# Gathered rows in a ring of two, one transpose per tile for four matmuls, in a top-32 attention and two-layer mixture-of-experts kernel

## The chip, the cores and the metric

One Trainium2 chip, one core of it. The metric is device time in microseconds (us) of one execution of the whole program. Three runs of the kernel before gave 1107.25, 1108.45 and 1108.89 us; the median, 1108.45 us, is what the change is measured against. Engine names: PE is TensorE's matmul, PEld its weight load, DVE is VectorE, ACT is ScalarE, POOL is GpSimd, SP is SyncE (it issues DMAs here).

## The reference

Three layers run one after the other. The change touches only the last one.

```python
# 1. attention over (4, 8, 576, 64): scores, only the 32 largest of a row are kept, softmax, times v
# 2. soft mixture of experts on x = (2304, 512): 8 experts with 4 slots each
#    d = softmax(x @ phi, over tokens); slot_out = relu((d.T @ x) @ w1[e]) @ w2[e]
#    x = softmax(x @ phi, over slots) @ slot_out            # every row is a mix of 32 rows
# 3. top-2 mixture of experts on that x
logits = x @ w_gate
noisy_logits = logits + np.log1p(np.exp(x @ w_noise)) * noise
top2 = np.argpartition(-noisy_logits, 2, axis=1)[:, :2]
top2_w = softmax of the two chosen logits
for e in range(8):
    for k in range(2):
        mask = top2[:, k] == e
        h = np.maximum(x[mask] @ w1[e], 0.0)                # 512 -> 1024
        out[mask] += top2_w[mask, k, None] * (h @ w2[e])    # 1024 -> 512
```

Since layer 2 makes each row of x a combination of 32 slot rows with weights c (one row of 32 numbers per token), the kernel never forms x for layer 3. It multiplies slot rows and w1 once per expert (a matrix `g_sb[e]`), and a token needs only its 32 combination weights, already scaled by its gate.

## The kernel before, in words

The first 780 us are attention, the soft layer and the routing. Routing ends with a table in DRAM, `xs_rows`: for each of the 4608 (token, choice) pairs a row of 32 numbers, and with a list in SBUF, `list_i`, which gives for each of up to 44 tiles of 128 pairs the row numbers to gather and the output rows to add to. The tiles are sorted by expert. With this input there are 40 tiles, five for most experts.

The last stage, from about 794 us, is a software pipeline over these tiles. Each engine runs a hardware loop per expert with bounds read from a table (`tile_bounds`), and semaphores tie the engines together. For tile i:

- POOL holds the indices of a tile in two small buffers `now[0]` and `now[1]` (`fetch`, line 1349, a copy of two numbers per partition: gather index and output index), gathers the 128 rows of 32 numbers from DRAM into the single buffer `x_in` (`gather`, line 1354, an indirect DMA) and adds the finished outputs to DRAM (line 1373, an indirect DMA with add). In one turn of its loop it fetches indices, waits for the output copy (`f_yc`), issues the scatter, waits until TensorE has read `x_in` (`f_t`), issues the gather, and then waits until the scatter has landed (`f_out`).
- PE, `f_trans` (line 776): four matmuls with `x_in` as 32 columns of weights and the identity as moving operand. They write the transposed rows four times, one above the other, into one PSUM bank. It waits for the gather (`x_ready`). This is done one tile ahead: it stands behind the first-layer matmuls of the tile before.
- ACT, `c_high` (line 947) copies that bank to `cs`, rounded to fp32r, and DVE, `c_low` (line 1233) turns the lower half of `cs` into the rounding remainder.
- PE, line 794: eight matmuls of `g_sb[e]` and `cs` (layer one of the expert). ACT, line 960: two Relu into `h_hi`. DVE, line 1250: the remainder `h_lo`.
- PE, lines 805 and 810: 16 and 8 matmuls with 512 columns each (layer two), with `w2_hi`, `w2_lo` and `h_hi`, `h_lo`. The first of them waits for the Relu (`f_hc`) and for `f_yc`, that is until DVE has copied the output of the tile before out of the bank (line 1237).
- Between experts ACT makes `w2_high` of the weights of a coming expert (line 926, two instructions), DVE makes `w2_low` (line 1207, two instructions), and ACT issues the DMA that loads 2 MB of weights for experts 4 to 7 (line 375, at the start of experts 1 to 4). Behind the first expert ACT also copies `g_sb` 6 and 7 (line 920).

Each engine executes its own queue in order, so the order of the work is what the loops write down, and an instruction that waits holds back all behind it on its engine.

## Time and profile before

| | us |
|---|---|
| median of the three runs | 1108.45 |
| the profiled execution | 1109.94 |
| its span | 1108.1 |
| PE busy | 939.6 (85%) |
| ACT busy | 617.3 (56%) |
| DVE busy | 817.3 (74%) |
| POOL busy | 708.6 (64%) |
| 40 turns of the tile loop | about 794 to 1108.1 |

The profiled execution took 1.5 us more than the median of the others. The busy shares are averages over stages with different limits: in the first 750 us DVE, ACT and POOL are busy together, and in the last 310 us PE is busy nearly all the time while the others have long gaps. The profile's chain of waits says the same for its last stretch: it runs along PE, lines 805, 810, 794 and 776, with breaks at a few places.

### The profile page before, as it was taken

What the parts mean: (1) busy time and instruction counts of PE and PEld (TensorE: products, weight loads), DVE (VectorE), ACT (ScalarE), POOL (GpSimd) and SP (SyncE); (2) the same over time, 40 slices, a digit from 0 to 9 for tenths busy, and PEclk for the clock granted to TensorE, in tenths of its full rate; (3) what the DMA queues carried; (4) which work ended last, traced back from release to release, by engine and by line L of the source; (5) the groups of instructions that cost most, each with busy time, mean ns of one, the idle gap of its engine ahead of it and who ended that gap; (6) DMA issues with size and microseconds to landing.
All of it is one profiled execution on the core that took longest, in us unless ns stands there. A gap on an engine that the chain in (4) does not pass through costs nothing.

```text
span 1108.1 us, 20890 instructions
## 1 busy us (share of the span) xinstructions
PE 939.6 (85%) x6032; PEld 639.7 (58%) x6032; DVE 817.3 (74%) x1870; ACT 617.3 (56%) x1199; POOL 708.6 (64%) x900
## 2 busy tenths in 40 slices
PE   3888888888888888888888897865699999899995
PEld 1655555555555555555555574222387787788884
DVE  6999999999999999999999964008525442444331
ACT  5888887788878877878888841102414331231110
POOL 2798989899899899899899851002234344344443
PEclk9999999999999999999999988966899999899998
DMA  9911011011011011011001007899524534433332
GB/s 352 390 46 35 11 45 44 0 44 44 0 44 44 0 44 44 0 44 44 30 14 44 0 1 290 351 421 425 236 30 106 116 50 104 109 40 40 40 41 31
DMA packets 21585, 105.12 MB, mean 95 GB/s; under 512 B 2944, under 2 KB 4016, under 8 KB 12464
## 3 DMA queue, kind: packets, MB, share of 16 engines
q1 hardware_dynamic: 13696, 84.54, 19.4%
q0 software_dynamic: 7136, 11.20, 7.7%
q10 hardware_dynamic: 720, 8.98, 2.2%
q8 instruction: 17, 0.28, 0.1%
q14 instruction: 16, 0.13, 0.0%
HBM read 88.37 MB, written 16.07 MB: 94 GB/s over the span
## 4 chain that ended last, share of the span: by engine, by line
DVE 39%; PE 29%; issue 22%; DMA 5%; ACT 2%; DVEq 2%; POOL 1%; SPq 0%; ACTq 0%; POOLq 0%; PEldq 0%
PE psum L805 12%; DVE arena L996 10%; DVE arena L1003 8%; PE psum L810 5%; DVE arena L992 5%; DVE arena L1009 3%; DVE arena L980 3%; DVE arena L984 2%; DMA arena<-w_soft 2%; DVE arena L988 2%; PE psum L794 2%; DMA arena<-xs_rows,arena 2%; DVE arena L1000 2%; DVE w_lo L1207 1%; PE psum L523 1%
## 5 line engine op out<-in xcount | busy, mean ns | idle before, releaser
L1289 POOL TENSOR_SCALAR arena<-arena 128x576 bf16<-128x576 f32 x142 | 246.7, 1738 | 55.4 <-DVE arena L1009 27.9
L564 PE MATMUL psum<-arena 128*128 128x130 f32 (+3 forms) x1600 | 227.9, 284 | 0.2 <-ACT arena L855 0.2
L564 PEld LDWEIGHTS psum<-arena 128*128 128x128 f32 (+3 forms) x1600 | 187.3, 180 | 43.2 <-ACT arena L855 13.6
L523 PE MATMUL psum<-arena 64*128 64x288 f32 (+1 forms) x640 | 112.0, 461 | 98.2 <-DVE arena L988 93.8
L1298 POOL TENSOR_TENSOR arena<-arena 128x576 f32<-128x576 f32 x142 | 178.6, 1277 | 0.0
L960 ACT ACTIVATE h_hi<-psum 128x512 fp32r<-128x512 f32 x80 | 43.6, 596 | 217.6 <-PE psum L794 217.6
L836 ACT ACTIVATE arena<-psum,arena 128x576 bf16<-128x576 f32 x144 | 106.6, 740 | 91.7 <-DVE arena L980 91.7
L1237 DVE COPY arena<-psum 128x512 f32 x41 | 28.3, 691 | 166.9 <-PE psum L810 156.6
L805 PE MATMUL psum<-w_hi,h_hi 128*128 128x512 f32 x320 | 135.6, 424 | 5.5 <-DVE arena L1237 2.8
L805 PE MATMUL psum<-w_lo,h_hi 128*128 128x512 f32 x320 | 130.0, 406 | 0.0
L523 PEld LDWEIGHTS psum<-arena 64*128 64x128 f32 (+1 forms) x640 | 44.3, 179 | 146.5 <-DVE arena L988 119.8
L839 ACT ACTIVATE arena<-arena 128x576 bf16<-128x576 bf16 x144 | 111.6, 775 | 4.7
L984 DVE MAX8 arena<-psum 128x8 f32<-128x576 f32 x144 | 108.8, 755 | 5.9 <-PE psum L535 5.8
L846 ACT ACTIVATE arena<-arena 128x576 f32<-128x576 f32 x144 | 112.2, 779 | 0.0
L829 ACT COPY arena<-psum 128x576 f32<-128x576 f32 x144 | 91.7, 637 | 35.9 <-PE psum L523 35.9
L1373 POOL DMA_INDIRECT out<-arena x40 | 63.8, 1595 | 73.7 <-PE psum L776 69.6
L1003 DVE MAX8 arena<-arena 128x8 f32<-128x576 f32 x144 | 107.2, 745 | 0.0
L988 DVE MATCH_REPLACE8 arena<-arena,psum 128x576 f32<-128x576 f32 x144 | 106.8, 741 | 0.0
L980 DVE MAX8 arena<-arena 128x8 f32<-128x576 f32 x144 | 106.0, 736 | 0.1
L992 DVE MAX8 arena<-arena 128x8 f32<-128x576 f32 x144 | 106.0, 736 | 0.0
L996 DVE MATCH_REPLACE8 arena<-arena 128x576 f32<-128x576 f32 x144 | 106.0, 736 | 0.0
L550 PE MATMUL psum<-arena 128*128 128x128 f32 x576 | 92.0, 284 | 2.8 <-POOL arena L1298 2.8
(192 smaller groups left out, 1602.8 us busy)
## 6 DMA issues: line engine op xcount, KB each, us to landing
weights<-w_soft SPq DMA_DIRECT2D x21, 1024.0 KB, 17.0
arena<-qkv SPq DMA_DIRECT2D x15, 1189.0 KB, 5.3
weights<-w_top SPq DMA_DIRECT2D x12, 1024.0 KB, 27.2
arena<-w_soft SPq DMA_DIRECT2D x11, 1024.0 KB, 12.1
weights<-w_top SPq DMA_DIRECT2D x3, 2048.0 KB, 18.9
weights<-w_top ACTq DMA_DIRECT2D x3, 2048.0 KB, 7.7
out<-arena SPq DMA_DIRECT2D x1, 4864.0 KB, 18.3
arena<-w_top SPq DMA_DIRECT2D x4, 1024.0 KB, 27.7
```

What stands on the lines that cost most here:

```text
L523: last = nc.tensor.matmul(bank(2 * (t % 2) + x, SH)[q0:q0 + rows, :], qT[u][half, w * P + q0:w * P + q0 + rows], kT[u][half, h * SH:(h + 1 ...
L564: last = nc.tensor.matmul(o_place(n, k)[0:rows, :], wT[0:kr, t % 2, kc, q0:q0 + rows], v_, start=(kc == 0), stop=(kc == KC - 1))
L805: nc.tensor.matmul(bank(B_Y), h_hi[:, f, :], w[:, f, :], start=(f == 0 and part_ == 0), stop=False)
L846: nc.scalar.activation(e_sb[t % S_SLOTS], s_sb[t % S_SLOTS], ACT.Exp, bias=nmax[n % 3][:, x:x + 1], scale=SCALE).then_inc(expd, 1)
L980: nc.vector.max(top(t, 0), s_sb[t % S_SLOTS]).then_inc(top8, 1)
L984: nc.vector.max(top(t, 1), scores_of(t)).then_inc(top16, 1)
L988: nc.vector.match_replace(by_half(work[t % 2]), top(t, 1), scores_of(t), NEG).then_inc(struck16, 1)
L992: nc.vector.max(top(t, 2), work[t % 2]).then_inc(top24, 1)
L996: nc.vector.match_replace(work[t % 2], top(t, 2), work[t % 2], NEG).then_inc(struck24, 1)
L1003: nc.vector.max(top(t, 3), work[t % 2]).then_inc(top32, 1)
L1289: nc.gpsimd.tensor_scalar(keep[t % 2], s_sb[t % S_SLOTS], kth_sb[:, t % S_SLOTS:t % S_SLOTS + 1], None, ALU.is_ge) \
L1298: nc.gpsimd.tensor_tensor(e_sb[t % S_SLOTS], e_sb[t % S_SLOTS], keep[t % 2], ALU.mult) \
```

## The change

The gather gets a ring of two buffers, `x_ring`, instead of `x_in`, and POOL runs it four tiles ahead of the output instead of three (`AHEAD = 4`). The gather and output indices sit in separate buffers (`nowx`, `nowo`), so POOL makes two small copies per tile, one in front of the scatter and one between scatter and gather. A new ACT instruction, `x_copy`, waits for the gathered rows and copies them four times side by side into a 128x128 tile `x_cur`; PE's `f_trans` is one transpose of `x_cur`. The gather now waits for `x_c` (ACT has read the ring buffer) and for the gather before it to land (`x_ready`), no longer for `f_t`. The list of tiles is one column longer (48 for 47).

```diff
--- before.py
+++ after.py
@@ -61,7 +61,8 @@
 TILES = 2 * N // P + E
 ROWS = 2 * N
-COLS = TILES + 3
+AHEAD = 4
@@ -134,7 +135,7 @@
         list_f = take(2 * COLS)
         list_at = at[0] - 2 * COLS
         list_i = list_f.bitcast(I32).rearrange("p (n v) -> p n v", v=2)
-        now = [take(2).bitcast(I32) for _ in range(2)]
+        nowx, nowo = [[take(1).bitcast(I32) for _ in range(2)] for _ in range(2)]
         tab = take(32).bitcast(I32)
         tiny = take(64)
 
...
-         x_in, _, _) = lay(
+         x_ring, _, _) = lay(
-            DC * P, 2 * E, WE // 4, SL, 8, P)
+            DC * P, 2 * E, WE // 4, 2 * SL, 8, P)
...
@@ -195,6 +196,7 @@
         logit = logit_f.rearrange("p (t s) -> p t s", t=TT)
         ed = ed_f.rearrange("p (t s) -> p t s", t=TT)
         cw = logit
+        x_cur = logit_f[:, 0:P]
         cT = cT_f.rearrange("p (b q) -> p b q", b=5)
         soT = soT_f.rearrange("p (c s) -> p c s", c=DC)
         so4 = so4_f.rearrange("p (c r s) -> p c r s", c=DC, r=4)
...
@@ -770,19 +773,16 @@
                 g_stack(e)
 
 
-            def f_trans(need):
-                pe.wait_ge(x_ready, need)
-                for r in range(4):
-                    last = nc.tensor.matmul(bank(B_X, P)[32 * r:32 * r + 32, :], x_in[:, 0:SL], ident,
-                                            start=True, stop=True, skip_group_check=True)
-                last.then_inc(f_t, 1)
+            def f_trans(n):
+                pe.wait_ge(x_c, n + 1)
+                nc.tensor.transpose(bank(B_X, P), x_cur, ident).then_inc(f_t, 1)
 
             pe.wait_ge(rt_ready, 1)
             bounds = tile_bounds(pe)
             pe.sem_inc(f_y, 1)
             pe.wait_ge(g_ev[0], 6)
             pe.wait_ge(g_ev[1], 6)
-            f_trans(16)
+            f_trans(0)
             for e in range(E):
                 t0, t1 = bounds[e], bounds[e + 1]
                 pe.wait_ge(w_lo, 2 * e + 2)
@@ -795,7 +795,7 @@
                                                 start=True, stop=True)
                         if f % 4 == 3:
                             last.then_inc(f_h, 1)
-                    f_trans(16 * i + 32)
+                    f_trans(i + 1)
                     pe.wait_ge(f_yc, i + 1)
 
                     for f in range(FC):
@@ -810,10 +810,6 @@
                         last = nc.tensor.matmul(bank(B_Y), h_lo[:, f, :], w2_hi[e % 4][:, f, :],
                                                 start=False, stop=(f == FC - 1))
                     last.then_inc(f_y, 1)
-            tl = bounds[E]
-            for n in range(2):
-                hold(pe, x_ready, 16 * tl + 16 * n + 32)
-                pe.sem_inc(f_t, 1)
 
 
         @block.scalar
@@ -948,7 +944,14 @@
 
             act.wait_ge(rt_ready, 1)
             bounds = tile_bounds(act)
+            def x_copy(n, slot):
+                act.wait_ge(x_ready, 16 * n + 16)
+                nc.scalar.copy(x_cur.rearrange("p (r s) -> p r s", r=4),
+                               slot.unsqueeze(1).broadcast_to([P, 4, SL])).then_inc(x_c, 1)
+
+            x_copy(0, x_ring[:, 0:SL])
             c_high(1)
+            x_copy(1, x_ring[:, SL:2 * SL])
             for e in range(E):
                 t0, t1 = bounds[e], bounds[e + 1]
                 if 0 < e <= 4:
@@ -961,12 +964,16 @@
                                              bank(B_H + x).rearrange("p (f q) -> p f q", f=4), ACT.Relu) \
                             .then_inc(f_hc, 1)
                     c_high(i + 2)
+                    x_copy(i + 2, x_ring[:, bass.ds((i + 2) % 2 * SL, SL)])
                 if e == 0:
                     g_out(6)
                     g_out(7)
                     w2_high(2)
                 if e < E - 3:
                     w2_high(e + 3)
+            hold(act, x_ready, 16 * bounds[E] + 48)
+            hold(act, x_c, bounds[E] + 2)
+            act.sem_inc(x_c, 1)
 
 
         @block.vector
...
@@ -1345,39 +1352,44 @@
                                     cst[:, C_PICK:C_PICK + PICKS].unsqueeze(2).broadcast_to([P, PICKS, COLS]),
                                     ALU.mult).then_inc(hot_pool, 1)
 
-            def fetch(n, slot):
-                nc.gpsimd.tensor_copy(now[slot], list_i[:, bass.ds(n, 1), :].rearrange("p n v -> p (n v)")) \
-                    .then_inc(idx_set, 1)
-                hold(pool, idx_set, n + 1)
+            def fetch(to, n, v, ready, count):
+                nc.gpsimd.tensor_copy(to, list_i[:, bass.ds(n, 1), v]).then_inc(ready, 1)
+                hold(pool, ready, count + 1)
 
             def gather(slot):
                 nc.gpsimd.indirect_dma_start(
-                    x_in, None, xs_dram[:, :], bass.IndirectOffsetOnAxis(ap=now[slot][:, 0:1], axis=0),
+                    x_ring[:, slot * SL:slot * SL + SL], None, xs_dram[:, :], bass.IndirectOffsetOnAxis(ap=nowx[slot], axis=0),
                     bounds_check=ROWS + P - 1, oob_is_err=True).then_inc(x_ready, 16)
 
             pool.sem_inc(out_free, 3)
             pool.wait_ge(idx_ready, 2)
             pool.wait_ge(tabled, 16)
-            fetch(0, 1)
-            gather(1)
+            for n in range(2):
+                fetch(nowx[n], n, 0, idx_x, n)
+                if n > 0:
+                    pool.wait_ge(x_ready, 16 * n)
+                gather(n)
             pool.wait_ge(rt_ready, 1)
             pairs = pool.value_load(tab[0:1, E + 1:E + 2], min_val=1, max_val=TILES // 2)
-            for n in range(1, 3):
-                fetch(n, (n + 1) % 2)
-                pool.wait_ge(f_t, n)
-                gather((n + 1) % 2)
+            for n in range(2, AHEAD):
+                pool.wait_ge(x_c, n - 1)
+                fetch(nowx[n % 2], n, 0, idx_x, n)
+                pool.wait_ge(x_ready, 16 * n)
+                gather(n % 2)
             with pool.Fori(0, pairs) as i:
                 for k in range(2):
-                    fetch(2 * i + k + 3, k)
+                    fetch(nowo[k], 2 * i + k + AHEAD, 1, idx_o, 2 * i + k)
                     hold(pool, f_yc, 2 * i + k + 2)
                     nc.gpsimd.indirect_dma_start(
-                        out[:, :], bass.IndirectOffsetOnAxis(ap=now[k][:, 1:2], axis=0), y_sb[k], None,
+                        out[:, :], bass.IndirectOffsetOnAxis(ap=nowo[k], axis=0), y_sb[k], None,
                         bounds_check=N + P - 1, oob_is_err=True, compute_op=ALU.add).then_inc(f_out, 16)
-                    hold(pool, f_t, 2 * i + k + 3)
+                    hold(pool, x_c, 2 * i + k + AHEAD - 1)
+                    fetch(nowx[k], 2 * i + k + AHEAD, 0, idx_x, 2 * i + k + AHEAD)
+                    hold(pool, x_ready, 32 * i + 16 * k + 16 * AHEAD)
                     gather(k)
                     pool.wait_ge(f_out, 32 * i + 16 * k + 16)
                     pool.sem_inc(out_free, 1)
-            hold(pool, x_ready, 32 * pairs + 48)
+            hold(pool, x_ready, 32 * pairs + 16 * AHEAD)
 
 
 def constants():
```

POOL's loop, one of its two halves, before. `indices` go by line 1349, the scatter is the DMA to `out`, the gather the DMA from `xs_rows`:

```order
L1349 COPY arena<-arena 128x2
L325 REGISTER_ALU
L325 REGISTER_ALU [waits idx_set]
L1373 DMA out<-arena 2432x512 [waits f_yc]
L1354 DMA arena<-xs_rows,arena 128x32 [waits f_t]
L1378 ISA
L1349 ISA [waits f_out]
```

The same half after the change (1356 is the index copy, 1383 the scatter, 1360 the gather):

```order
L1356 COPY arena<-arena 128x1
L328 REGISTER_ALU
L328 REGISTER_ALU [waits idx_out]
L1383 DMA out<-arena 2432x512 [waits f_yc]
L328 REGISTER_ALU
L1356 ISA [waits x_copied]
L1356 COPY arena<-arena 128x1
L328 REGISTER_ALU
L328 ISA [waits idx_x]
L1360 DMA arena<-xs_rows,arena 128x32 [waits x_ready]
L1390 REGISTER_ALU
L1356 ISA [waits f_out]
```

One index copy, with its own semaphore, has come between scatter and gather, and the gather waits for `x_copied` and `x_ready` where it waited for `f_t`.

ACT's loop of the first expert and what follows it, before (960 the Relu, 947 `c_high`, 920 the copies of `g_sb`):

```order
L960 ACTIVATE h_hi<-psum 128x512 [waits f_h]
L959 REGISTER_ALU
L960 ACTIVATE h_hi<-psum 128x512 [waits f_h]
L946 REGISTER_ALU
L947 CAST cs<-psum 128x128 [waits f_t]
L957 REGISTER_ALU
L957 COMPARE_AND_BRANCH
L920 CAST g_58<-psum 128x512 [waits g_rep]
L920 CAST g_59<-psum 128x512 [waits g_rep]
```

After (963 the Relu, 943 `c_high`, 949 the new `x_copy`):

```order
L963 ACTIVATE h_hi<-psum 128x512 [waits f_h]
L962 REGISTER_ALU
L963 ACTIVATE h_hi<-psum 128x512 [waits f_h]
L942 REGISTER_ALU
L943 CAST cs<-psum 128x128 [waits f_t]
L948 ISA
L949 ISA [waits x_ready]
L949 COPY arena<-arena 128x128
L960 REGISTER_ALU
L960 COMPARE_AND_BRANCH
L916 CAST g_58<-psum 128x512 [waits g_rep]
L916 CAST g_59<-psum 128x512 [waits g_rep]
```

The copy, with its wait for the gathered rows, stands behind `c_high` and ahead of all that ACT does between two experts.

PE's loop of the first expert up to the second layer, before (794 layer one, 776 `f_trans`):

```order
L794 MATMUL psum<-cs,g_52 128x128 [waits f_c]
L794 MATMUL psum<-cs,g_52 128x128 x7
L774 ISA
L776 MATMUL psum<-arena 32x128 [waits x_ready]
L776 MATMUL psum<-arena 32x128 x3
L803 ISA [waits f_yc]
L805 MATMUL psum<-w_hi_67,h_hi 128x512 [waits f_hc]
```

After (778 is `f_trans`):

```order
L794 MATMUL psum<-cs,g_52 128x128 [waits f_c]
L794 MATMUL psum<-cs,g_52 128x128 x7
L777 REGISTER_ALU
L778 MATMUL psum<-arena 128x128 [waits x_copied]
L803 ISA [waits f_yc]
L805 MATMUL psum<-w_hi_67,h_hi 128x512 [waits f_hc]
```

The transpose keeps the place of the four matmuls, and its wait is on ACT's copy; the waits on `f_yc` and `f_hc` stay right behind it.

## Rows read from the trace of the kernel before

**Rows 1.** Busy time of each engine in one stretch: us, then instructions in brackets.
```profile
core 0: us, PE busy (x) PEld busy (x) DVE busy (x) ACT busy (x) POOL busy (x), PEclk, DMA share, GB/s
970.90:1089.00 118.10, 118.00 (x676) 95.66 (x672) 47.50 (x72) 24.52 (x54) 50.84 (x51) 1.00 0.32 40
```

**Rows 2.** Waits of PE, 800 to 1108.1 us: total us, times, longest.
```profile
PE psum L776 <- DMA arena<-xs_rows,arena: 6.3, 4, 2.6
...
PE psum L805 <- ACT h_hi L960: 2.6, 2, 2.2
```

**Rows 3.** Instructions in time, one undisturbed tile: start, us, what, [idle before].
```profile
1018.50 1.00 PE L794 MATMUL psum<-cs,g 128*128 128x128 f32 x8
...
1018.95 0.69 DVE L1237 COPY arena<-psum 128x512 f32 x1 [4.62 <-PE psum L810]
1019.09 1.08 ACT L960 ACTIVATE h_hi<-psum 128x512 fp32r<-128x512 f32 x2 [5.76 <-PE psum L794]
...
1019.43 0.42 PE L776 MATMUL psum<-arena 128*32 128x128 f32 x8
...
1019.78 0.19 PEld L805 LDWEIGHTS psum<-w_hi,h_hi 128*128 128x128 f32 x1 [0.20 <-ACT h_hi L960]
...
1020.06 0.27 ACT L947 CAST cs<-psum 128x128 fp32r<-128x128 f32 x1
...
1025.48 1.00 PE L794 MATMUL psum<-cs,g 128*128 128x128 f32 x8
```

**Rows 4.** Instructions in time, two of the tiles that waited for their rows.
```profile
885.09 0.43 PE L776 MATMUL psum<-arena 128*32 128x128 f32 x8 [1.11 <-DMA arena<-xs_rows,arena]
...
885.44 0.19 PEld L805 LDWEIGHTS psum<-w_hi,h_hi 128*128 128x128 f32 x1 [0.20 <-issue]
...
960.91 0.65 PE L776 MATMUL psum<-arena 128*32 128x128 f32 x8 [2.60 <-DMA arena<-xs_rows,arena]
```

**Rows 5.** Chain of waits, layer two of three tiles: start, us, what.
```profile
922.19 5.43 PE psum L805 x16
...
961.56 6.30 PE psum L805 x16
...
970.93 3.93 PE psum L805 x16
```

**Rows 6.** Instructions of PE in time, attention: four transposes in a row.
```profile
400.53 0.60 PE L550 MATMUL psum<-arena 128*128 128x128 f32 x4
```

**Rows 7.** Instructions of POOL and DVE in time, gathers and scatters.
```profile
774.23 0.18 POOL L1349 COPY arena<-arena 128x2 int32<-128x2 int32 x1 [6.79 <-DVE arena L1222]
775.34 1.30 POOL L1354 DMA_INDIRECT arena<-xs_rows,arena  x1 [0.93 <-POOL arena L1349]
...
886.69 1.59 POOL L1373 DMA_INDIRECT out<-arena  x1 [1.08 <-issue]
...
1020.57 1.59 POOL L1373 DMA_INDIRECT out<-arena  x1 [1.50 <-PE psum L776]
...
1021.37 4.50 DVE L1207 TENSOR_TENSOR w_lo<-arena,w_hi 128x2048 fp32r<-128x2048 f32 x2
...
1022.47 2.14 POOL L1354 DMA_INDIRECT arena<-xs_rows,arena  x1 [0.31 <-issue]
```

**Rows 8.** From issue to landing: the gather (line 1354), then the scatter (line 1373).
```profile
DMA to landing us min/median/max: 2.3/3.4/7.0
...
DMA to landing us min/median/max: 4.6/4.8/8.7
```

**Rows 9.** Instructions in time at the start of the stage (ACT, DVE).
```profile
794.08 0.27 ACT L947 CAST cs<-psum 128x128 fp32r<-128x128 f32 x1 [0.17 <-PE psum L776]
...
795.59 0.29 DVE L1233 TENSOR_TENSOR cs<-psum,cs 64x128 fp32r<-64x128 f32 x1 [2.32 <-issue]
```

**Rows 10.** Instructions of ACT in time, between experts 0 and 1, then 3 and 4.
```profile
832.89 3.75 ACT L926 CAST w_hi<-weights 128x2048 fp32r<-128x2048 f32 x2
...
840.10 1.12 ACT L960 ACTIVATE h_hi<-psum 128x512 fp32r<-128x512 f32 x2
...
944.71 3.74 ACT L926 CAST w_hi<-weights 128x2048 fp32r<-128x2048 f32 x2
...
950.44 0.34 ACTq L375 DMA_DIRECT2D arena<-w_top  x1
```

**Rows 11.** Instructions of POOL in time at the end of the program.
```profile
1097.97 1.60 POOL L1373 DMA_INDIRECT out<-arena  x1 [1.53 <-PEq L816]
1099.87 1.07 POOL L1354 DMA_INDIRECT arena<-xs_rows,arena  x1 [0.31 <-issue]
```

8 lines of the change are left out of this document (5 added, 3 removed).

## The prediction

> **What bounds the kernel now.** I read the page first: all that the change touches lies in the last stage, from 794 us, so the table of busy time by stretch comes next. Between 970.9 and 1089.0 us PE is busy 118.00 of 118.10 us at full granted clock, while DVE, ACT and POOL are busy 47.5, 24.5 and 50.8 us [rows 1]. PE is the bound there, and a cheaper engine elsewhere is worth nothing. Second, the list of PE's waits: in the whole stage it stood idle four times for gathered rows, 6.3 us together, and twice for a late Relu, 2.6 us [rows 2]. Third, one undisturbed tile in order of time [rows 3]. A tile takes 1025.48 - 1018.50 = 6.98 us. The reader is to see what ends just before layer two starts at 1019.78: PE's four replication matmuls (from 1019.43), the first Relu, and DVE's output copy. Fourth, two of the waiting tiles [rows 4] and the length of layer two behind such waits [rows 5].
>
> **Part 1, four matmuls become one transpose: 0.** The group of line 776 holds PE from 1019.43 to 1019.78, 0.35 us, also where no Relu is late: 885.09 to 885.44 [rows 3, 4]. In attention, four transposes take 0.60 us with the tail of the last one [rows 6], so one costs at most 0.15 us of PE. By busy time 0.20 us per tile and 8 us over 40 tiles would go. But two other releases fall on the same instant. The first Relu starts at 1019.09 and takes 1.08/2 = 0.54 us by the row, and the row's own weight load of layer two at 1019.78 names ACT as its releaser [rows 3]. DVE's copy runs from 1018.95 for 0.69 us, to 1019.64 [rows 3], plus the semaphore. Both start from layer one and the end of layer two, which the change leaves alone. If the Relu's semaphore arrives right at its end (1019.63) and the copy's (1019.64) too, 0.14 us per tile could be had, 5.6 us over 40; if either is what releases 1019.78, nothing. Below nothing there is no reason, as the transpose waits for a copy made five microseconds earlier. The named releaser decides: I take 0, with 5.6 us kept as the other end.
>
> **Part 2, rows gathered further ahead: -10.2 us.** The four idle times go: 6.3 us [rows 2]. Behind two of them PE came back at half clock. Layer two's first 16 matmuls took 5.43 us at 922 and 6.30 us at 961 against 3.93 us at 970.93 [rows 5], which is 1.5 + 2.4 = 3.9 us; the other two waits (1.11 us at 885 [rows 4] and the fourth, which is what is left of the 6.3) are left at their bare length. Without an idle PE the clock should not fall, so 6.3 + 3.9 = 10.2 us. The clock's share is the less certain one; if it stays, 6.3 us.
>
> Is something else late in place of the rows? In the new order the gather stands behind an extra index copy. Behind a scatter comes the next POOL instruction after 0.31 us [rows 7], the copy takes 0.18, and from a copy's end to the gather that uses it 0.93 us pass [rows 7]: 1.42 us for 0.31, so the gather is issued 1.1 us later in its turn. Its turn is counted from the scatter, 1020.57 - 1018.50 = 2.07 us behind the tile's start [rows 3, 7]. So the gather starts 2.07 + 1.59 + 1.42 = 5.1 us into a tile and lands at 8.5 us with the median of 3.4 us [rows 8], 1.5 us into the next tile. ACT wants it behind `c_high`, at 1020.33 - 1018.50 = 1.8 us [rows 3]: no wait. With the longest landing, 7.0 us [rows 8], it lands 5.1 us into the tile; ACT copies it until about 5.4 and has to be free for the next Relu at 6.98 + 0.59 = 7.6 us. So 2.2 us are to spare even then.
>
> POOL can be held up on top. Beside DVE's `w2_low` the gather took 2.14 us for the usual 1.07 [rows 7], and it now has one more instruction there; each of DVE's two lasts 2.25 us, which would eat the 2.2 us at the boundaries between experts where a 2 MB load runs. The Trainium skill says so too (GPSIMD Engine Reference, Key points): GpSimd shares its SBUF interfaces with VectorE and contends with DVE instructions that read two SBUF inputs. By that rule, the trace agrees at 2.14 us. I put 0.3 us for the four boundaries with a load (0 to 2 us).
>
> The Trainium skill has another figure for a GpSimd DMA (DMA: Bandwidth & Descriptors, Anatomy of one DMA): about 2.0 us plus bytes over 436 GB/s, which for the 16 KB of a gather would be 2.04 us and leave ACT never waiting. The trace's 3.4 and 7.0 us are longer, and the sum goes by them.
>
> **Part 3, the ACT copy.** No row shows a 128x128 copy from SBUF to SBUF on ACT. The nearest is `c_high`, the same shape out of PSUM, 0.27 us [rows 3]; the far end is half of a `w2_high` pair, 1.9 us for sixteen times the columns [rows 10], which bounds it well. I take 0.3 us with its register work (0.12 to 0.6). Inside an expert ACT is idle 5.7 us per tile [rows 3], which hides it. Between experts:
> - 0 to 1: ACT copies `g_sb` and makes two `w2_high` without a break, from before 832.89 until the Relu at 840.10 [rows 10], and PE waits for that Relu, 2.2 us [rows 2]. Here the copy is paid in full, 0.3 us, and a longer idle time can lengthen the stretch at half clock by as much: +0.7 us (0.3 to 3, if the copy also waits for a late gather).
> - 1 to 4: `w2_high` ends at 944.71 + 3.74 = 948.45, and ACT then waits until it may issue the load at 950.44 [rows 10]. That is a cover of 2.0 us less the issue itself, so 0.3 us costs nothing; if the gather is late, see above.
>
> **Part 4, the first tile: 0.** PE's replication of tile 0 is now behind ACT's copy: copy, transpose, `c_high` in a line instead of `c_high` alone at 794.08 [rows 9]. That adds about 0.3 + 0.15 us and two semaphores, and `c_high` ends near 795.2. DVE's `c_low` started at 795.59 for its own reasons (it had been idle for 2.32 us with nothing to wait for [rows 9]). Hidden; +0.5 us as the other end.
>
> **Part 5, the last turn: +1.1 us.** The last scatter starts at 1097.97 and the last, unused gather at 1099.87 [rows 11]. With 4.8 and 3.4 us [rows 8] they land at 1102.8 and 1103.3, so the gather ends the program. It moves by the 1.1 us above. If the scatter's landing is what counts, 0.6.
>
> The longer list adds two columns to 36 small matmuls and about 2% to two index operations: under 0.1 us.
>
> **Sum:** 0 - 10.2 + 0.3 + 0.7 + 0 + 1.1 = -8.1 us. On the profiled execution, 1109.94 us (span 1108.1 plus 1.8 around it), that is 1101.8. The median of the runs shown is 1.5 us lower, 1108.45, and from it the sum gives 1100.4 us.
>
> **Rivals.**
> - *PE gets its 0.14 us per tile as well.* For: Relu and copy end by the rows at 1019.63 and 1019.64. Against: the row at 1019.78 names ACT. 1100.4 - 5.6 = 1094.8 us.
> - *The stalls go but come back as late Relus.* ACT's `x_copy` waits for the gather ahead of the Relu and of `w2_high`, beside the 2 MB loads. For: landing 7.0 us at worst, POOL held by DVE. Against: the 2.2 us computed. If each of the three stalls beside a load keeps half of its length and the clock its drop: -10.2 + 2.7 + 3.9 + 2.1 = -1.5, 1107.0 us.
> - *POOL's turn becomes the period: slower.* POOL still waits for the scatter's landing in each turn: 4.8 + 0.18 + 1.08 us until the next scatter [rows 7, 8] make 6.06 us, and PE's turn is 6.98. It decides from a landing of 5.7 us on. The extra copy and the gather (1.59 + 1.42 + 1.07 = 4.1 us) fit inside the landing; if the landing is counted behind the gather, or the later gather delays the scatter, 4.8 becomes 5.9 and more. At 6.2 us each of some 35 tiles costs 0.5 us: +17 - 8.1, 1117 us. Against: nothing in the rows couples the scatter's landing to a gather behind it.
> - *The change doesn't do what it says:* the rows still come late. It would need a landing of 9 us; the longest is 7.0 [rows 8]. 1108 us.
>
> **How the numbers follow.** Forecast 0.64 (own range 1097.5 to 1104.5, with the clock's 3.9 us kept or not and the boundary up to 2 us worse), PE gain 0.12, late Relus 0.13, POOL's turn 0.07, no effect 0.04. Three runs of this kernel spread by 1.6 us, so 0.2%, 2.2 us, is what can be told from no change. Late Relus fall half into "within 0.2%" (up to 1106.2 counts as faster) and more: 0.09 of 0.13; with no effect 0.04 that is 0.13; slower 0.07; faster 0.80. Range for 8 in 10: from 1096.0 (part of the PE gain) to 1106.5.
>
> **What would show it.** Right: no wait of PE for rows or for the new ACT copy beyond 0.3 us; a tile of 6.9 to 7.0 us as before, with layer two's first weight load still released by ACT or DVE; POOL's gather 1.4 us behind the scatter; PE's wait for the Relu at the first boundary 2.5 to 3 us; half-speed layer two only there and at the stage's start; the last gather 3.0 us behind the last scatter. Wrong: tiles of 6.85 us or less without a wait (part 1), idle PE in front of the Relu at later boundaries (late Relus), a period above 7.1 us with DVE waiting for `out_free` (POOL's turn).

## The result, and the profile after

The changed kernel took 1096.5 us (median of 6 runs, 1094.6 to 1102.6), the kernel before 1107.9 us beside it on the same chip (6 runs, 1106.0 to 1109.2). The ratio is 0.9907 [0.9879, 0.9936]. (The ratios here are taken over the runs and differ a little from the quotients of the medians.) Forecast were 1100.4 us and a range of 1096.0 to 1106.5, so the median lies near the lower end of that range, and 1.0 us below the forecast's own range of 1097.5 to 1104.5. Two later comparisons of the same two kernels gave less: 0.9967 [0.9951, 0.9982] and 0.9946 [0.9925, 0.9967]. So the gain is real, but the medians differed by 4.2 to 11.4 us, and why it varies is part of what had to be explained.

The page of the changed kernel begins so (span, then busy time of each engine):

```profile
span 1093.4 us, 20681 instructions
...
PE 922.1 (84%) x5745; PEld 628.4 (57%) x5745; DVE 817.3 (75%) x1870; ACT 627.0 (57%) x1241; POOL 723.6 (66%) x942
```

Its own time is 1095.2 us, the span 14.7 us less than the 1108.1 of before. The first step is to cut that span where the first and where the last of the 40 tiles starts its layer one (the lines L794). The change touches what lies between, and the tail. All times are us, in profiled executions:

| execution | first tile starts | to the start of the last tile (39 turns, "the loop") | rest |
|---|---|---|---|
| before, first | 795.94 | 291.96 | 20.2 |
| before, again | 796.52 | 286.59 | 20.2 |
| changed, first | 790.79 | 282.85 | 19.8 |
| changed, again | 790.02 | 282.87 | 19.6 |
| changed, third | 797.42 | 282.42 | 19.7 |

Some 5.1 of the 14.7 us lie in front of the stage, 9.11 in the loop, 0.5 behind it. The 5.1 us are not the change's. The stage starts near 790 us in some executions and near 796 us or later in others, and either code has shown both: the changed kernel began at 797.42 us in its third execution, and the version with the gather first (below), which has the code of before up to the stage, at 790.10. The early and the late executions already differ between 640 and 660 us. Busy time there, before and after the change (the third number from the end of a row is the granted clock):

```profile
640.00:660.00 20.00, 18.23 (x136) 15.09 (x135) 14.99 (x35) 10.33 (x21) 11.58 (x19) 0.83 0.01 1
640.00:660.00 20.00, 17.02 (x148) 13.63 (x146) 15.01 (x35) 10.32 (x22) 11.10 (x19) 1.00 0.01 2
```

It is 0.83 in the three late executions of the table and 1.00 in the two early ones and in the version with the gather first. What makes it fall there in some executions was not settled.

**Inside the stage, PE's waits for rows are gone.** Waits from 795 to 1094 us (engine, line waited for, total us, times, longest), to be read against [rows 2]:

```profile
ACT arena L949 <- DMA arena<-xs_rows,arena: 26.9, 14, 5.7
...
POOL arena L1360 <- DMA arena<-xs_rows,arena: 10.7, 3, 4.1
PE psum L805 <- ACT h_hi L963: 4.2, 5, 2.7
```

No row says that PE waited for `xs_rows`. The landing now reaches ACT, which waited for it 14 times and 26.9 us, and POOL, which waited 10.7 us for an earlier gather to land. PE hardly noticed: of its 4.2 us for a Relu, 2.67 are the first boundary's. The chain of waits gives layer two's length, to be held against [rows 5]. At the stage's start (6.64 us) and behind the first boundary, where one expert's tiles end and the next one's begin, it is long, and the granted clock is 0.50 from 836.2 to 839.0 us. In all later tiles it is 3.9 to 4.0 us:

```profile
836.17 5.51 PE psum L805 x16
844.66 4.00 PE psum L805 x16
...
922.14 3.92 PE psum L805 x16
```

**An undisturbed tile is as long as before, 1018.37 - 1011.39 = 6.98 us.** Instructions in time (start, us, what, [idle before]), the counterpart of [rows 3]:

```profile
1011.39 1.01 PE L794 MATMUL psum<-cs,g 128*128 128x128 f32 x8
1011.84 0.69 DVE L1244 COPY arena<-psum 128x512 f32 x1
1011.98 1.09 ACT L963 ACTIVATE h_hi<-psum 128x512 fp32r<-128x512 f32 x2 [5.53 <-PE psum L794]
...
1012.23 0.29 PE L778 MATMUL psum<-arena 128*128 128x128 f32 x1
...
1012.66 0.19 PEld L805 LDWEIGHTS psum<-w_hi,h_hi 128*128 128x128 f32 x1 [0.33 <-ACT h_hi L963]
...
1013.94 1.60 POOL L1383 DMA_INDIRECT out<-arena  x1 [1.02 <-issue]
...
1014.29 0.30 ACT L949 COPY arena<-arena 128x128 f32 x1 [1.06 <-DMA arena<-xs_rows,arena]
...
1016.76 1.07 POOL L1360 DMA_INDIRECT arena<-xs_rows,arena  x1 [1.02 <-issue]
...
1018.37 1.01 PE L794 MATMUL psum<-cs,g 128*128 128x128 f32 x8
```

Layer two's first weight load stood 1.28 us behind the tile's start in [rows 3] and stands 1.27 us behind it now; only the idle time in front of it grew from 0.20 to 0.33 us. PE's busy time by stretch shows the same over 17 tiles (us, then busy us of PE, PEld, DVE, ACT, POOL, granted clock):

```profile
965.00:1082.60 117.60, 113.40 (x549) 92.32 (x547) 46.43 (x71) 27.07 (x66) 56.68 (x69) 1.00 0.33 40
```

In [rows 1] PE was busy 118.00 of 118.10 us; now it lacks 4.20 us, 0.25 per tile, for the same length of tile. What the transpose saved became idle time of PE.

**The gather.** It is issued 16.76 - 13.94 = 2.82 us behind the scatter's start, 1.22 behind its end. From issue to landing, the gather of line 1360 and the scatter of line 1383, for [rows 8]:

```profile
DMA to landing us min/median/max: 2.4/2.6/8.3
...
DMA to landing us min/median/max: 4.7/4.8/7.4
```

The median of the gather fell from 3.4 to 2.6 us, its maximum rose. The worst three lie beside the second, third and fourth of the 2 MB loads. At 871.58 is the second:

```profile
867.19 4.49 DVE L1214 TENSOR_TENSOR w_lo<-arena,w_hi 128x2048 fp32r<-128x2048 f32 x2
867.48 2.05 POOL L1356 COPY arena<-arena 128x1 int32 x1
870.55 2.08 POOL L1360 DMA_INDIRECT arena<-xs_rows,arena  x1 [1.03 <-issue]
...
871.58 0.35 ACTq L378 DMA_DIRECT2D weights<-w_top  x1
...
878.46 1.00 PE L794 MATMUL psum<-cs,g 128*128 128x128 f32 x8
...
879.05 0.30 ACT L949 COPY arena<-arena 128x128 f32 x1 [5.70 <-DMA arena<-xs_rows,arena]
...
879.74 1.07 POOL L1360 DMA_INDIRECT arena<-xs_rows,arena  x1 [4.09 <-DMA arena<-xs_rows,arena]
880.04 0.50 PE L805 MATMUL psum<-w_hi,h_hi 128*128 128x512 f32 x1 [0.30 <-ACT h_hi L963]
```

Beside DVE's `w2_low` the index copy in front of the gather ended at 869.53, 1.5 us behind the scatter (866.40 + 1.61); in an undisturbed tile it ends 0.2 us behind it. The gather then took 8.3 us to land. The rows came so late that ACT's copy began at 879.05, the moment at which the Relu was due (in an undisturbed tile it starts 0.59 us behind the tile's start). ACT waited 5.7 us, and the tile became 0.3 us longer. Before, late rows held up PE itself, at this load for 1.11 us [rows 4].

**The last turn,** for [rows 11]. POOL:

```profile
1082.60 1.60 POOL L1383 DMA_INDIRECT out<-arena  x1 [1.62 <-ACTq L976]
...
1085.42 1.07 POOL L1360 DMA_INDIRECT arena<-xs_rows,arena  x1 [1.02 <-issue]
```

The unused gather stands 2.82 us behind the last scatter, where it stood 1.90.

### The profile page after: what moved, and what is told of

It reads as the page before. It is cut to its first block, busy times and chain, and to the rows that moved or that the text cites. A ratio compares the mean times of both kernels' runs of the same rounds, so it can differ in the third digit from the quotient of the medians.

```text
span 1093.4 us, 20681 instructions
## 1 busy us (share of the span) xinstructions
PE 922.1 (84%) x5745; PEld 628.4 (57%) x5745; DVE 817.3 (75%) x1870; ACT 627.0 (57%) x1241; POOL 723.6 (66%) x942
## 3 DMA queue, kind: packets, MB, share of 16 engines
q1 hardware_dynamic: 13696, 84.54, 19.7%
## 4 chain that ended last, share of the span: by engine, by line
DVE 39%; PE 29%; issue 22%; ACT 4%; DMA 3%; DVEq 2%; POOL 1%; ACTq 0%; SPq 0%; POOLq 0%
PE psum L805 14%; DVE arena L1003 10%; DVE arena L1010 8%; PE psum L810 6%; DVE arena L999 5%; DVE arena L1016 3%; DVE arena L987 3%; DVE arena L991 2%; DVE arena L995 2%; DMA arena<-w_soft 2%; ACT h_hi L963 2%; DVE arena L1007 2%; PE psum L794 1%; PE psum L705 1%; PE psum L526 1%
## 5 line engine op out<-in xcount | busy, mean ns | idle before, releaser
L567 PE MATMUL psum<-arena 128*128 128x130 f32 (+3 forms) x1600 | 225.6, 282 | 0.3 <-ACT arena L851 0.2
L567 PEld LDWEIGHTS psum<-arena 128*128 128x128 f32 (+3 forms) x1600 | 185.1, 178 | 43.4 <-ACT arena L851 13.8
L805 PE MATMUL psum<-w_hi,h_hi 128*128 128x512 f32 x320 | 132.7, 415 | 12.2 <-ACT h_hi L963 4.2
```

What stands on the lines that cost most here:

```text
L567: last = nc.tensor.matmul(o_place(n, k)[0:rows, :], wT[0:kr, t % 2, kc, q0:q0 + rows], v_, start=(kc == 0), stop=(kc == KC - 1))
L805: nc.tensor.matmul(bank(B_Y), h_hi[:, f, :], w[:, f, :], start=(f == 0 and part_ == 0), stop=False)
```

## The experiments

### The same kernels again

Two points were open: is 9 us of the loop the normal gain, and does the start of the stage depend on the kernel?

> The changed kernel itself, as the yardstick for the others of this call. Theory A (the stalls for rows are gone, the rest of a tile is as it was): ratio to the kernel before 0.989 to 0.993, that is 8 to 12 us less. Theory B (part of the first result was a lucky stretch before 790 us, where the two profiles already differ by 5.2 us): the part from the first layer-one matmul of the stage to its last is 9 us shorter again, and what lies before it differs from the kernel before by less than 3 us.

Measured: 1097.16 us against 1101.99 (8 and 19 runs), ratio 0.9967 [0.9951, 0.9982], outside what was expected. The profiled loop, 282.87 us, is again 9 us shorter than that of the first trace of before, but the stage began 6 us earlier than there, where less than 3 was expected.

> The kernel before once more, for a second trace, since its runs spread from 1099.7 to 1108.8 us in the last comparison. Theory A (its time depends on how many of the waits for rows there are and whether the clock falls behind them): the waits for rows differ from the first trace's 6.3 us in number or length, and the sum of waits and half-clock stretches accounts for the difference in time within 2 us. Rival (the spread comes from before 790 us): the waits in the last stage are the same as in the first trace.

Measured: 1105.19 us in one run, span 1103.4. PE's four waits of that execution:

```profile
885.60 0.43 PE L776 MATMUL psum<-arena 128*32 128x128 f32 x8 [1.04 <-DMA arena<-xs_rows,arena]
...
921.83 0.43 PE L776 MATMUL psum<-arena 128*32 128x128 f32 x8 [1.18 <-DMA arena<-xs_rows,arena]
...
958.73 0.42 PE L776 MATMUL psum<-arena 128*32 128x128 f32 x8 [1.96 <-DMA arena<-xs_rows,arena]
...
1085.03 0.43 PE L776 MATMUL psum<-arena 128*32 128x128 f32 x8 [0.92 <-DMA arena<-xs_rows,arena]
```

They sum to 5.1 us, and behind none of them did PE come back at half clock: the two tiles that were 10.14 and 12.27 us long in the first execution are 8.11 and 9.01 here. The loop is 286.59 us, 3.7 more than the changed kernel's 282.87. Three of the four waits lie in it, 5.1 - 0.92 = 4.2 us. The changed kernel gives 0.4 us of that back in the first tile (13.67 for 13.31) and 0.3 at the first boundary, and gains 0.2 elsewhere. The first execution's loop is another 5.4 us longer: 1.1 of waiting, 3.9 of half clock in layer two [rows 5], and 0.4 elsewhere, more than half of it the slower matmuls of line 776 in one tile (0.65 us for 0.42).

> The changed kernel again, as the yardstick for this call. Theory A (the gain over the kernel before is some 4 us of bare waits and tail, and a further 4 us in those executions in which the clock fell behind a wait): ratio 0.991 to 0.997. Rival (the first comparison's 0.991 holds everywhere): 0.989 to 0.993.

Measured: 1099.49 us against 1103.68 (11 and 16 runs), ratio 0.9946 [0.9925, 0.9967]. Its profiled stage began at 797.42 us, later than in either trace of before, and its loop took 282.42. The same 64 matmuls in the chains in front of the stage, in the first execution of before, then in the changed kernel's first:

```profile
689.97 8.81 PE psum L683 x64
```

```profile
688.52 7.12 PE psum L686 x64
```

In the changed kernel's third execution they take 8.81 us again, 1.7 us more than in its first, and with the code of before they also took 7.12 us, in the version with the gather first. The 5.1 us in front of the stage in the first comparison are of that kind. The mean granted clock of a run goes with its time: of the 19 runs of before in the first of these two comparisons, twelve at 0.968 to 0.971 took 1099.7 to 1104.7 us and three at 0.960 took 1108.3 to 1108.8; the changed kernel took 1094.3 to 1097.8 us in six runs at 0.967 to 0.970 and 1099.1 and 1100.5 in two at 0.964 and 0.963.

### Four matmuls in place of the transpose

```diff
-                nc.tensor.transpose(bank(B_X, P), x_cur, ident).then_inc(f_t, 1)
+                for r in range(4):
+                    last = nc.tensor.matmul(bank(B_X, P)[32 * r:32 * r + 32, :], x_cur[:, 0:SL], ident,
+                                            start=True, stop=True, skip_group_check=True)
+                last.then_inc(f_t, 1)
```

> The changed kernel with the one transpose undone: four matmuls read the first 32 columns of the copied tile, ring, copy and order of the gathers stay. Theory A (the cheaper PE work fills a gap that Relu and output copy leave anyway): the period of an undisturbed tile stays 6.97 to 6.99 us and the time equals the changed kernel's within 2 us. Rival (PE's 0.2 us per tile are part of the gain): 8 us slower than the changed kernel, a tile of 7.15 us or more.

Measured: 1098.25 us, ratio to before 0.9957 [0.9936, 0.9978], beside 0.9967 of the changed kernel in the same comparison. The tile is 6.99 us for 6.975, the loop 284.86 for 282.85. Of these 2.0 us, 1.3 are one longer first boundary (12.28 us for 11.01), behind a wait of 2.40 us that is shorter than the changed kernel's 2.67, and 0.9 one tile in which PE waited 0.56 us for ACT's copy. The transpose is worth 0.6 us over 40 tiles at most, and no difference of the two kernels' times can be told.

### What hides the transpose

My reading was that the Relu releases layer two. Each Relu was cut in two, and PE waits for quarters:

```diff
-                        if f % 4 == 0:
-                            pe.wait_ge(f_hc, 2 * i + f // 4 + 1)
+                        if f % 2 == 0:
+                            pe.wait_ge(f_hc, 4 * i + f // 2 + 1)
...
-                    for x in range(2):
-                        act.wait_ge(f_h, 2 * i + x + 1)
...
+                    for x in range(4):
+                        act.wait_ge(f_h, 2 * i + x // 2 + 1)
```

> The changed kernel with each of the two Relu of a tile cut in two (256 columns each); layer two waits for the quarter it needs. In the changed kernel's trace layer two starts 0.08 us behind the first Relu's end and 0.13 us behind the output copy's. Theory A (the Relu is released last, the output copy 0.05 us before it): an undisturbed tile falls from 6.975 to 6.92 to 6.94 us, some 2 us over the stage. Rival (the Relu alone bounds it, the copy is far off): the whole gap goes and a tile falls to 6.7 us.

Measured: 1096.28 us, ratio 0.9939 [0.9915, 0.9963], and the tile stays at 6.975 us. Both numbers of the expectation failed. The tile in time:

```profile
1014.62 1.00 PE L794 MATMUL psum<-cs,g 128*128 128x128 f32 x8
...
1015.08 0.69 DVE L1244 COPY arena<-psum 128x512 f32 x1
1015.21 1.21 ACT L963 ACTIVATE h_hi<-psum 128x256 fp32r<-128x256 f32 x4 [5.51 <-PE psum L794]
...
1015.89 0.19 PEld L805 LDWEIGHTS psum<-w_hi,h_hi 128*128 128x128 f32 x1 [0.33 <-ACT h_hi L963]
```

By the row's 1.21 us for four quarters, the first is ready about 0.3 us behind 1015.21, yet the weight load still starts 1.27 us behind the tile, and its row still names ACT. What ends just before it is DVE's output copy, 1015.08 + 0.69 = 1015.77. Then the copy alone was shortened, and then both:

```diff
-                nc.vector.tensor_copy(y_ring[:, bass.ds((i + 1) % 2 * D, D)], bank(B_Y)).then_inc(f_yc, 1)
+                nc.vector.tensor_copy(y_ring[:, bass.ds((i + 1) % 2 * D, D // 2)], bank(B_Y, D // 2)).then_inc(f_yc, 1)
```

(Half of each output row keeps what an earlier tile left.)

> The changed kernel with half of the output copy (256 of 512 columns; the other half of each output tile is left out). Theory A (Relu last): the period of a tile stays 6.97 us. Rival (output copy last): it falls by 0.05 us or more.

> Relu cut in two and half of the output copy left out, together. Theory A (Relu and output copy end within 0.05 us of each other and together hide PE's transpose): only now does PE's own work set the tile: 6.65 to 6.75 us. Rival (something else holds layer two back at that instant): 6.9 us or more.

Measured, in one run each: the half copy alone 1097.17 us and a tile of 6.945 us; both together 1087.29 us and a tile of 6.73 us. With the half copy (first fence) the weight load starts 1.24 us behind the tile, with both (second) 1.02:

```profile
1013.96 1.01 PE L794 MATMUL psum<-cs,g 128*128 128x128 f32 x8
1014.41 0.42 DVE L1244 COPY arena<-psum 128x256 f32 x1
...
1015.20 0.19 PEld L805 LDWEIGHTS psum<-w_hi,h_hi 128*128 128x128 f32 x1 [0.30 <-ACT h_hi L963]
```

```profile
1012.73 1.00 PE L794 MATMUL psum<-cs,g 128*128 128x128 f32 x8
...
1013.57 0.29 PE L778 MATMUL psum<-arena 128*128 128x128 f32 x1
1013.75 0.19 PEld L805 LDWEIGHTS psum<-w_hi,h_hi 128*128 128x128 f32 x1
```

So the order is: copy last, the Relu 0.03 us ahead of it, and PE's own work 0.22 us ahead of both. Taking away either one gives 0.03 us or nothing; both give 0.245 us per undisturbed tile. The loop fell by less than 40 times that, from 282.85 to 276.02 us, that is by 6.8: one tile took 8.32 us, in which PE waited 1.30 us for ACT's copy of the rows, and the first boundary stayed at 11.19.

### ACT's copy without the ring

One buffer for the gathered rows, three tiles ahead as before, with ACT's fourfold copy and the transpose kept; the gather waits for ACT's copy. Against the changed kernel, in excerpts:

```diff
-                    x_ring[:, slot * SL:slot * SL + SL], None, xs_dram[:, :], bass.IndirectOffsetOnAxis(ap=nowx[slot], axis=0),
+                    x_in, None, xs_dram[:, :], bass.IndirectOffsetOnAxis(ap=now[slot][:, 0:1], axis=0),
...
-                    fetch(nowo[k], 2 * i + k + AHEAD, 1, idx_o, 2 * i + k)
+                    fetch(2 * i + k + 3, k)
...
-                    hold(pool, x_c, 2 * i + k + AHEAD - 1)
-                    fetch(nowx[k], 2 * i + k + AHEAD, 0, idx_x, 2 * i + k + AHEAD)
-                    hold(pool, x_ready, 32 * i + 16 * k + 16 * AHEAD)
+                    hold(pool, x_c, 2 * i + k + 3)
```

> The other part alone: one buffer, three tiles ahead as before, but ACT copies the rows and PE transposes once. Theory A (the ring's extra tile of distance is what takes the waits away, and the copy needs it): ACT waits for a gather that starts 3.96 us into a tile and lands at 7.4 us, is late for the Relu due at 7.6 us, by 0.1 to 0.3 us in each tile and by 3 us or more at each boundary where it also makes w2_high: 15 to 30 us slower than before. Rival (the transpose brings the gain, the ring little): 3 to 8 us faster than before.

Measured: 1132.13 us, ratio 1.0279 [1.0257, 1.0301]. Its waits from 790 to 1131 us:

```profile
ACT arena L947 <- DMA arena<-xs_rows,arena: 213.5, 41, 6.9
...
PE psum L803 <- ACT h_hi L961: 26.4, 17, 8.1
```

ACT waits for the rows in every tile, but inside an expert that mostly costs PE nothing or 0.3 us. The loss is at five boundaries, where ACT makes `w2_high` behind the late copy and ahead of the Relu: PE waits 8.1 us there once and 3.8 us four times, and the tiles are 12.2 to 16.8 us long. It is the second rival of the prediction, in full. The copy without the ring costs some 30 us; it is the second buffer, with the tile of distance that it allows, that buys the cover. The ring without ACT's copy was not run.

### The gather ahead of the scatter

Here the kernel before was changed: POOL waits for the transpose and gathers first, and scatters behind it.

```diff
+                    hold(pool, f_t, 2 * i + k + 3)
+                    gather(k)
...
-                    hold(pool, f_t, 2 * i + k + 3)
-                    gather(k)
```

> The kernel before with two lines moved: in each turn POOL issues the gather ahead of the scatter, still one buffer, four matmuls, no copy. Theory A (the rows came late only because the gather stood behind the scatter, on POOL and in its DMA queue): the four waits for rows vanish or fall below 0.5 us together, the half-clock stretches behind them too, so 8 to 11 us faster than before, like the changed kernel. Rival (one buffer is too few: the transfer itself takes up to 7 us beside a 2 MB load): the three waits at those loads stay at half their length or more, and the gain is under 5 us.

Measured: 1146.98 us against 1101.99, ratio 1.0409 [1.0389, 1.043], where I had expected a gain. PE waited 32.3 us in 16 places for rows. POOL in time:

```profile
1018.14 0.19 POOL L1349 COPY arena<-arena 128x2 int32 x1 [3.51 <-DMA out<-arena]
1019.29 1.08 POOL L1354 DMA_INDIRECT arena<-xs_rows,arena  x1 [0.95 <-POOL arena L1349]
1020.67 1.60 POOL L1375 DMA_INDIRECT out<-arena  x1 [0.31 <-issue]
...
1026.13 0.18 POOL L1349 COPY arena<-arena 128x2 int32 x1 [3.86 <-DMA out<-arena]
```

One turn is 1026.13 - 1018.14 = 7.99 us: copy 0.19, 0.95 to the gather, gather 1.08, 0.31 to the scatter, and 5.46 from the scatter's issue to the copy that waits for its landing. PE's tile is 6.98 us, so POOL sets the period; with the turns beside the loads its 39 turns take 8.3 us on average (first scatter at 807.4, last at 1130.7). This is the slower rival ("POOL's turn becomes the period") made real, at 8.0 us, and by another way than priced there: not a later landing but the gather and its 0.95 us in front of the scatter. The changed kernel is spared it because its gather and the 1.2 us in front of it stand behind the scatter, inside the landing.

### Two ACT copies

A second copy per tile, ahead of the one that counts, into columns that nothing reads:

```diff
+                nc.scalar.copy(logit_f[:, P * (1 + n % 2):P * (2 + n % 2)].rearrange("p (r s) -> p r s", r=4) if isinstance(n, int) else
+                               logit_f[:, bass.ds(n % 2 * P + P, P)].rearrange("p (r s) -> p r s", r=4),
+                               slot.unsqueeze(1).broadcast_to([P, 4, SL]))
```

> The changed kernel with a second, unused copy of the gathered rows on ACT in each tile, 0.3 to 0.4 us more there. Theory A (the copy costs only where ACT has no gap, at the first boundary): an undisturbed tile stays at 6.97 us, the boundary tile behind expert 0 grows from 11.0 by 0.3 to 0.5 us, and no other boundary by more than 0.1. Rival (ACT's copy delays the pipeline in each tile): 0.1 us or more per tile.

Measured: 1102.41 us in one run, undisturbed tiles 6.97 us. The first boundary took 12.43 us for 10.8 to 11.0, with PE's wait 2.86 us and a longer stretch at half clock behind it (layer two in the chain, against 5.51 above; the granted clock is 0.50 from 841.7 to 846.0 us):

```profile
841.63 6.73 PE psum L805 x16
```

The 0.3 us copy is free in an undisturbed tile. In the tile behind the second load, whose rows are late, it wasn't: 7.95 us for 7.28 to 7.37, where at most 0.1 more was expected. The first boundary was 1.4 to 1.6 us longer, most of it half clock. That the copy caused this is not shown: four matmuls in place of the transpose had as long a boundary (12.28 us) behind a shorter wait (2.40 us).

### The first boundary: `w2_high` of expert 2 behind tile 0

At the first boundary ACT has `w2_high` of expert 2 in front of the Relu. It was moved behind tile 0, with DVE's `w2_low`:

```diff
+                if e == 0:
+                    tile(0, x_ring[:, 0:SL])
+                    w2_high(2)
+                    t0 = 1
...
-                    w2_high(2)
```

> The changed kernel with the weights of expert 2 prepared (by ACT and DVE) behind tile 0 instead of behind expert 0, where ACT now works without a break and PE waits 2.7 us for it and restarts at half clock; for an input whose first expert has at least two tiles. Theory A (that boundary costs 4.0 us over a usual tile, and the ACT copy paid in full there is part of it): the boundary tile falls from 11.0 to 7.0 to 7.6 us, 3.5 to 4 us less than the changed kernel. Rival (the half clock is due to the load of 2 MB or comes anyway): the boundary tile stays above 8.5 us.

Measured: 1093.84 us (6 runs, 1091.6 to 1096.9) against 1103.68, ratio 0.9915 [0.9885, 0.9944]; the changed kernel in the same comparison had 0.9946. At the first boundary, 839.67 - 832.46 = 7.21 us:

```profile
832.46 1.01 PE L794 MATMUL psum<-cs,g 128*128 128x128 f32 x8
...
833.97 0.50 PE L805 MATMUL psum<-w_hi,h_hi 128*128 128x512 f32 x1 [0.37 <-ACT h_hi L955]
...
839.67 1.01 PE L794 MATMUL psum<-cs,g 128*128 128x128 f32 x8
```

That is 3.8 us of one tile, and the loop fell from 282.85 to 279.38; tiles with late rows gave 0.2 and 0.4 us of it back (7.48 and 7.37 us for 7.28 and 6.98). It has the lowest median of all versions that compute the whole, though its interval and the changed kernel's overlap.

### The loads issued by SP

On top of that, the four 2 MB loads inside the experts moved from ACT's queue to SP's:

```diff
+            firsts = [sp.value_load(tab[0:1, e:e + 1], min_val=min(e, 1), max_val=TILES) for e in range(5)]
+            for e in range(1, 5):
+                hold(sp, f_y, firsts[e] + 1)
+                load_w2t(sp, e + 3)
...
-                if 0 < e <= 4:
-                    hold(act, f_y, t0 + 1)
-                    load_w2t(act, e + 3)
```

> As the version with early weights, and the four 2 MB loads of experts 4 to 7 are issued by SP instead of ACT. Theory A (the Relu behind such a load is 0.2 to 0.35 us late because ACT first waits for layer two and issues the DMA): the four boundary tiles fall from 7.15 to 7.35 us to 6.98 to 7.05 us, about 1 us less in all. Rival (they are late because the gather's copy waits beside the load): no change.

Measured: 1095.59 us (6 runs, 1090.6 to 1097.3), ratio 0.9909 [0.9876, 0.9942]. The four boundary tiles at a load, 7.21, 7.15, 7.04 and 7.16 us in the version before, are 6.98, 6.97, 6.87 and 7.06 us, and the tile behind the second load, late by its rows, stayed at 7.48: two delays with two causes. The loop, 277.91 us, is the shortest of the complete versions. In the time it can't be told from the version before it, since its six runs spread by 6.7 us: two at a mean granted clock of 0.972 took 1090.6 and 1090.7 us, four at 0.964 or 0.965 took 1095.6 to 1097.3.

## Why the prediction was right, and where its steps were not

**Part 2, the rows further ahead: right for the trace from which it was read.** The six tiles at and behind the last three loads fell from 52.2 to 42.8 us together, and the tail lost its wait of 1.0: 10.4 us, what was lost beside the loads already taken off, where 10.2 less 0.3 were forecast. All four waits of [rows 2] are gone, and so is the half-clock length of [rows 5]. The two tiles that had them, 10.14 and 12.27 us, are 6.85 and 6.98 us now. "The clock's share is the less certain one; if it stays, 6.3 us" held in another way than meant: it is the kernel before that varies. In its second execution the waits were 5.1 us and the clock did not fall, and the loop's gain was 3.7 us. The clock's term belongs to the execution that the change is compared with.

**The step inside part 2 that failed: "no wait" of ACT and "2.2 us to spare".** ACT waited 14 times, up to 5.70 us. In an undisturbed tile the order of POOL was as computed (1.22 us behind the scatter for 1.42), and the median landing was shorter (2.6 us for 3.4; it was 2.5 also in the version whose gather stands ahead of the scatter). Beside the second load two terms were too small. The index copy took until 1.5 us behind the scatter beside DVE's `w2_low`, so the gather started 6.2 us into its tile for the computed 5.1; and it landed after 8.3 us, for 7.0. Together they use up more than the 2.2 us to spare, and the tile became the 0.3 us longer that are seen above. At the third and the fourth load ACT still had 0.64 and 0.26 us to spare. POOL itself then waited up to 4.09 us for the gather ahead of it, which I had not put into the turn. It was cheap because ACT has 5.5 us idle per tile. The gather itself took 2.08 us beside `w2_low`, as in [rows 7].

**Part 1, the transpose: 0, right, with half the reason.** The result is 6.98 us per tile as before and 0.25 us more idle time in it. The reason given, "the named releaser is ACT", doesn't hold: with Relus of half the length the row still names ACT and nothing moves, and with half of DVE's copy 0.03 us goes. A wait for two semaphores is shown as one of them. The other end, 5.6 us, was low for what the two hide together: with both shortened the loop lost 6.8.

**Part 3, the ACT copy: 0.32 us at the median for 0.3.** At the boundary between experts 0 and 1 the tile went from 10.67 us (before, again: 10.69) to 11.01 and 10.80, that is +0.1 to +0.3 for a forecast +0.7. PE's wait there was 2.67 us, as forecast "2.5 to 3". That a longer wait lengthens the half-clock stretch is not borne out: layer two was as long behind a wait of 2.40 us (6.81 us) as behind one of 2.86 (6.73), and 5.51 us behind 2.67.

**Part 4, the start of the first tile: 0, right.** In front of the first L794 PE waits for DVE's `c_low` as before, but 0.66 us shorter (1.91 in the kernel before), which is what copy and transpose put in front of it:

```profile
790.79 1.97 PE L794 MATMUL psum<-cs,g 128*128 128x128 f32 x8 [1.25 <-DVE cs L1240]
```

Another 1.25 us would have been covered. The first tile itself took 13.68 us for 13.32, with a longer layer two, but this goes with the early start and not with the change: it was 13.29 us in the changed kernel's third execution, and 13.69 in the version with the gather first.

**Part 5, the tail: +0.3 to +0.5 us for +1.1.** The tail of before held a wait for rows of 1.01 us, which went, so that it is 0.5 us shorter as it stands and 0.5 longer without that wait (+0.3 between the second executions). The gather came 0.9 us later behind the scatter, and its landing was shorter.

**What the sum did not have.** It gave -8.1 us; the profiled stage has -9.6, the profiled span -14.7 and the first comparison's medians -11.4. What the sum lacks is the stretch in front of the stage: 5.1 us of the profiled span, which belong to no part and to neither kernel. The two later comparisons (4.8 and 4.2 us) gave about half of the sum. There most executions of before probably had no fall of the clock in the loop; the only such trace, of a run beside a third comparison, has none. That these two things explain the whole spread was not shown: two executions of before and three of the changed kernel were profiled. So the mechanism of part 2 was right, and the size of its clock term held for the execution that it was read from. That the first comparison's gain came out above the sum, with the median still inside the range by 0.5 us, is luck as far as the sum goes.

**Rivals.** "PE gets its 0.14 us per tile" is out: the tile is 6.98 us. "Late Relus" and "POOL's turn becomes the period" are both real mechanisms of this stage, as the version without the ring (+2.8%) and the one with the gather first (+4.1%) show, and the change misses both but for the 0.3 us beside a load: it puts the gather behind the scatter, and it puts a second buffer in front of ACT's copy. "The rows still come late" needed a landing of 9 us; the longest was 8.3. The same two facts that looked like details of the diff decide between 9 us gained and 30 to 45 us lost.

## What to carry to other kernels

When a buffer's wait stands on the bound engine, moving it to an engine with idle time is worth the wait and whatever the clock adds behind it; but the mover needs its own second buffer, or it passes the wait on. Price what a queue does in one turn, instruction by instruction and landing included, before you move anything ahead of a DMA whose landing the turn waits for. And where a piece of work of the bound engine is shortened without effect, shorten the others that end at the same instant together, not one by one: here neither of two was worth more than 0.03 us per tile alone, and both were worth 0.245.

## What the runs showed of the hardware

**The length of a wait didn't decide alone whether the clock fell.** The row of the first execution of before that isn't among [rows 4]:

```profile
921.77 0.43 PE L776 MATMUL psum<-arena 128*32 128x128 f32 x8 [1.62 <-DMA arena<-xs_rows,arena]
```

Before the change, the wait of 2.60 us at 961 [rows 4] and that of 1.62 us at 921.77 were followed by layer two at half clock, 6.30 and 5.43 us for 3.93 [rows 5], with a granted clock of 0.50 from 961.6 to 965.9 us; in the other execution waits of 1.96 and 1.18 us were not. At the first boundary waits of 2.2 to 2.9 us always were (5.3 to 6.8 us), and the 0.37 us there was not. Nor did the length of the wait decide how long the low clock lasted: in the version without the ring, four waits of 3.76 or 3.77 us were followed by layer two in 5.54, 5.55, 6.22 and 6.34 us.

**A gather's landing depends on what is in front of it in its queue and beside it.** The median was 3.4 us straight behind a scatter [rows 8], 2.6 us with 1.2 us between and 2.5 us ahead of the scatter; beside a 2 MB load it reached 7.0 before the change, 8.3 after it and 7.5 with the gather first. The Trainium skill (DMA: Bandwidth & Descriptors, Anatomy of one DMA) has about 2.0 us plus bytes over 436 GB/s; my estimate from it is 2.04 us for these 16 KB. The shortest landing here, 2.4 us, comes near to that figure, and the median of the changed kernel is 0.6 us above it.

**Matmuls of 512 columns at full granted clock came in two lengths.** In some tiles layer two took 3.92 us and the tile 6.85, in others 4.00 and 6.98, in both kernels and at a granted clock of 1.00. The short ones are the tiles of the fourth and the eighth expert, in every trace kept: their matmuls start 0.227 us apart, those of all other experts 0.233. These two experts share the buffers `w2_hi[3]` and `w2_lo[3]`, so it goes with these two buffers. What sets them apart was not tried.
